# Waiting on SyncE for the first w1 of an expert to land before the next expert's weights are sent

## The reference, cut to what matters

```python
x = attention(r, k, v, w, u)                 # 1536 rows of 384
for layer in (0, 1):                          # two mixtures of experts, E = 8, F = 1024
    logits = x @ w_gate (+ bias by modality in layer 0)
    e_idx  = argmax(logits)                   # one expert to a row
    gate   = softmax(logits) at e_idx
    for e in range(8):
        rows   = (e_idx == e)                 # layer 1: at most capacity = 384 of them
        out[rows] = gate[rows] * (relu(x[rows] @ w1[e]) @ w2[e])
    x = out                                   # w1[e]: 384 x 1024, w2[e]: 1024 x 384, float32
```

## Time and profile before

| what | us |
|---|---|
| median of 3 runs (394.46 to 395.70) | 395.65 |
| the profiled execution: time | 396.4 |
| the profiled execution: span | 394.3 |
| TensorE matmuls busy (3406) | 366.7 |
| VectorE busy | 209.6 |
| ScalarE busy | 133.0 |
| GpSimd busy | 184.5 |

### The profile page before, as it was taken

One profiled execution on the slowest core, in us unless ns is written; L12 is line 12 of the kernel. 1 busy time (PEld: TensorE's weight loads), 2 busy tenths in 40 slices (PEclk: granted clock), 3 DMA queues, 4 the chain that ended last, 5 costly groups with the idle time before them and its releaser, 6 DMA issues.

```text
span 394.3 us, 10784 instructions
## 1 busy us (share of the span) xinstructions
PE 366.7 (93%) x3406; PEld 356.9 (91%) x3407; DVE 209.6 (53%) x539; ACT 133.0 (34%) x230; POOL 184.5 (47%) x303
## 2 busy tenths in 40 slices
PE   4689999988999999999999999879999999999990
PEld 4579999977899999999999999769999999999990
DVE  4356666689688655555555577474214454244210
ACT  2447554410544222222222252105215555255220
POOL 6798999815455532323232334152434524444311
PEclk9999999998999999999999999699999999999996
DMA  6898774146999511111111321139349998492000
GB/s 128 142 353 185 164 161 100 40 129 169 402 405 404 215 40 40 40 40 40 40 40 40 112 114 40 13 82 403 122 153 350 317 327 299 136 345 98 27 23 17
DMA packets 68238, 62.08 MB, mean 157 GB/s; under 512 B 45493, under 2 KB 61028, under 8 KB 68080
## 3 DMA queue, kind: packets, MB, share of 16 engines
q1 hardware_dynamic: 63904, 51.26, 40.9%
q0 software_dynamic: 3744, 10.23, 7.9%
q10 hardware_dynamic: 560, 0.21, 0.2%
HBM read 52.85 MB, written 10.14 MB: 160 GB/s over the span
## 4 chain that ended last, share of the span: by engine, by line
PE 82%; DMA 6%; SPq 4%; DVE 3%; issue 2%; ACT 1%; POOL 1%; ACTq 0%; POOLq 0%; DVEq 0%
PE p_h L1203 35%; PE p_o L1225 28%; DMA w_sb<-in_moe_w 3%; PE p_sc L1118 3%; SPq L406 3%; PE p_x L1090 3%; PE p_xt L1180 2%; PE p_y L1100 2%; PE p_y L1106 2%; DMA w_raw<-in_moe_w 2%; PE p_kv L1081 1%; PE p_kt L1068 1%; PE p_rt L1072 1%; PE p_o L1050 1%; DMA xg<-x_rows,src_idx 1%
## 5 line engine op out<-in xcount | busy, mean ns | idle before, releaser
L1203 PE MATMUL p_h<-xT,w_sb 128*128 128x128 f32 x1296 | 149.3, 275 | 1.6 <-ACT xT L670 1.0
L1203 PEld LDWEIGHTS p_h<-xT,w_sb 128*128 128x128 f32 x1296 | 148.2, 192 | 2.3 <-issue 1.3
L982 DVE SCALAR_TENSOR_TENSOR h_lo<-p_h,h_hi 128x512 fp32r<-128x512 f32 x54 | 37.4, 692 | 78.9 <-ACT h_hi L753 77.8
L999 DVE CUSTOM_DVE_ANT_0 lg_prod<-y_row,wg_all 128x384 f32<-128x384 f32 x112 | 55.8, 554 | 41.9 <-ACT y_row L763 41.7
L1225 PE MATMUL p_o<-w_hi,h_hi 128*128 x216 | 75.4, 349 | 0.0
L1225 PE MATMUL p_o<-w_lo,h_hi 128*128 x216 | 73.1, 339 | 0.0
L1225 PE MATMUL p_o<-w_hi,h_lo 128*128 x216 | 73.0, 338 | 0.0
L753 ACT ACTIVATE h_hi<-p_h 128x512 fp32r<-128x512 f32 x54 | 32.3, 598 | 112.2 <-PE p_h L1203 112.2
L580 POOL TENSOR_TENSOR dst_mark<-zeros 128x1 f32<-128x1 f32 x54 | 15.7, 290 | 105.8 <-DVE y_row L999 68.6
L839 DVE TENSOR_TENSOR w_lo<-w_raw,w_hi 128x1024 fp32r<-128x1024 f32 x36 | 42.0, 1221 | 7.8 <-ACT w_hi L670 7.8
L580 POOL TENSOR_TENSOR src_mark<-zeros 128x1 f32<-128x1 f32 x54 | 18.8, 348 | 49.1 <-PE p_xt L1180 33.9
(11 more groups left out here) (183 smaller groups left out, 408.9 us busy)
## 6 DMA issues: line engine op xcount, KB each, us to landing
w_raw<-in_moe_w SPq DMA_DIRECT2D x12, 1536.0 KB, 9.7
w_sb<-in_moe_w SPq DMA_DIRECT2D x12, 1536.0 KB, 9.5
k_raw<-in_k SPq DMA_DIRECT2D x12, 192.0 KB, 3.2
r_raw<-in_r SPq DMA_DIRECT2D x12, 192.0 KB, 3.6
v_raw<-in_v SPq DMA_DIRECT2D x12, 192.0 KB, 3.8
x_rows<-x_rows SPq DMA_DIRECT2D x12, 192.0 KB, 1.9
out<-zeros SPq DMA_DIRECT2D x1, 2304.0 KB, 15.6
wg_all<-in_moe_w_gate_by_expert SPq DMA_DIRECT2D x1, 1536.0 KB, 6.6
```

The lines of the kernel that those rows point to most:

```text
L982: stt(h_lo[:, at, :], p_h[n][:, :, :], 0.0, h_hi[:, at, :].bitcast(F32), ALU.max, ALU.subtract).then_inc(h_ready[layer], 1)
L999: last = nv.tensor_tensor_reduce(out=lg_prod[:, n, :], in0=y_row[par][:, 0:DM], in1=wg2_all[:, e, :], op0=ALU.mult, op1=ALU.add, scale=1.0 ...
L1203: last = mm(p_h[half][:, f, :], w1_sb[place][:, c, col:col + P], xT[:, c, :], start=(c == 0), stop=(c == DC - 1))
```

## The change

In the branch `free < 1`, after w1 has been sent, SyncE waits until the semaphore of that place, `w1_loaded[place]`, has reached 16, which is the count that the first load ever into this place leaves when it has landed. Nothing else differs.

```diff
@@ -469,6 +469,7 @@
 
                                 expert_w2(place, read_layer, read_e)
                             expert_w1(place, read_layer, read_e)
+                            sp.wait_ge(w1_loaded[place], 16)
                         with sp.If(free > 0):
                             sp.wait_ge(w2_ready, NPC * (n - 1))
                             expert_w2(place, read_layer, read_e)
```

## The result

| | us |
|---|---|
| before, median of 4 runs (394.46 to 395.70) | 395.24 |
| changed, median of 4 runs (399.35 to 402.50) | 400.74 |
| ratio, 95% interval | 1.0121, 1.009 to 1.0153 |
| changed, profiled execution: time, span | 399.35, 397.3 |

The changed kernel is slower by 1.2%, some 4.8 us (3.6 to 6.0); the two medians themselves lie 5.5 us apart. The time lies in the range of the prediction, above its point of 398.9, and near rival A's 400.3.

What follows compares the result with a forecast made beforehand. TensorE, busy 366.7 of 394.3 us, was taken as the bound, so at most 0.7 us could be won. Forecast: median 395.65 + 3.2 us for tile 2's later start, clock loss 0, = 398.9 us; range 395.9 to 401.7.

Steps and rivals of the forecast that it cites:

- rival A: TensorE at tile 2: the forecast's wait plus idle time pulling the clock down, 1.4 us more, 400.3 us; chance 0.27.
- L (step d): Moment expert 2's w1 has landed in layer 0, releasing SyncE: stays at 107.7, so the 0.7 us aren't won.
- rival B: Shared queue: expert 2's w1 was slowed by loads behind it, so it lands at 105.4; 395.7 to 396.6 us; chance 0.18.
- (b): SyncE after release: expert 3's w2 goes out about 1.1 us later, w1 half a microsecond behind it.
- (c): Expert 3's two loads on idle DMA engines: 12.3 us from first issue to second landing, ends 11.0 and 13.3.
- (e): Expert 3's w1 lands at 121.1, 5.4 us later; less 2.2 us of room, tile 2's p_h starts 3.2 us later.
- The hole in the DMA rate: Sign to look for in the trace: a gap of about 2 us in the DMA rate after 107.7.
- (f): Expert 3's w2 lands about 6.8 us after issue, ScalarE waits 1.3 us; covered by tile 2's wait, cost 0.
- (g): Later loads: n = 3's w2 goes out near 110.6, lands at 125, wanted at 127.5; covered, as are those after.
- (h): TensorE's clock after 3.2 us idle before tile 2: loss taken as 0 in the forecast, 1.7 us as bound.
- C: Rival at layer 0's first tiles: faster by 0.7 us, 394.95, if both experts' w1 land early enough; chance 0.07.
- D: Rival: expert 3's pair and expert 4's w2 share the DMA engines evenly, delaying tile 2 some 4 to 6 us; chance 0.05.

Runs made afterwards that it cites:

- swap: Kernel before, but for n = 1 in layer 0 SyncE sends expert 2's w1 ahead of its w2, no wait added; ratio to before 1.0061.
- again3: The changed kernel run again unchanged, third repeat; ratio to before 1.0101.
- wait_w2: The changed kernel, but SyncE waits for expert 2's w2 instead of its w1; ratio to before 0.9976.
- hold_w1: Kernel before, with the wait for expert 2's w1 placed after sending expert 3's w2, before expert 3's w1; ratio to before 1.0019.
- again2: The changed kernel run again unchanged, second repeat; ratio to before 1.0147.
- again: The changed kernel run again unchanged, first repeat; ratio to before 1.0098.
- fill2: Second run of the changed kernel with 50 small filler matmuls on TensorE after tile 1 of layer 0; ratio to before 1.0067.
- fill: The changed kernel plus 50 small filler matmuls on TensorE after tile 1 of layer 0, within its wait; ratio to before 1.0085.
- wait_high6: The changed kernel, but SyncE is released when ScalarE has done the third piece of expert 2's w2; ratio to before 1.0136, 2 executions.

## Why the prediction was right, and where its size was off

**L (step d) held**, and with it rival B fell: expert 2's w1 took 11.82 us from its issue (11.8 to 12.7 in the four profiles). The reading behind it, that a load isn't slowed by one behind it on SyncE's queue and that some engines run ahead while the last one finishes, is borne out by swap and by the changed kernel, where 0.04 MB were left for the last 1.9 us. On B the prediction is not consistent: with 11.0 us for the pair its own sum puts tile 2 at 117.5, 0.4 us earlier than 117.89, where it writes 0; its "middle, 395.9" goes with the -0.4.

**SyncE's branches (b)**: 1.1 us was taken, 1.2 us is measured. **The pair (c)**: 12.3 us was taken; it was 12.1 in the first profile (110.50 to 122.56), and 11.5 to 11.6 in the other three. **The sum (e)**: 3.2 us later was forecast; the first profile has 3.2, the four together 2.7 to 3.6 (tile 2's start, from the issue of expert 2's w2), and executions with the filler give 3.1. The hole in the DMA rate was larger than the "about 2 us" that was to be looked for: 1.9 us before the landing and 3.7 behind it. It cost the sum nothing, as (c) counts from the issue.

**(f)** ScalarE waited 2.2 us for expert 3's w2, not 1.3, because this load took 7.6 us rather than 6.8; it was covered by the wait for w1, as said. **(g)** was off in a detail that cost nothing: the w2 of expert 4 went out 3.0 us after that of expert 3, not 1.8 (108.8 to 110.6), since the issue of the w1 between them took 0.9 us by itself; neither ScalarE nor TensorE had a further wait.

**(h) is the term that was mis-sized.** The forecast took 0 for the clock and gave 0.40 to that, 0.27 to rival A with 1.4 us. The runs show A's mechanism in two of four profiles of the changed kernel, at 1.6 and 2.9 us, and 1.3 us (0.3 to 2.4) in the mean of whole executions. The changed kernel's mean is 4.5 us above before, 3.1 for the wait and 1.3 for the clock, which lies at A's 4.65 rather than at the forecast's 3.25. The range held because it had been drawn to A's bound. The error was to treat the clock as a yes or no for the kernel; the profiles show it one way in two executions and the other way in two, so that a share of it belongs in the sum. The two rows, one with the loss and one without, said as much, and 0.27 x 1.4, or 0.4 us, is what the prediction's own chance would have put in. The bound of 1.7 us was too low as well: in again3 the clock was at 0.50 from 120 to 126 us, longer than the 4 us of that row.

**C** (faster) fell, as L didn't move and no pair after empty engines took less than 11.5 us. **D** (all three share, 4 to 6 us) fell too: expert 3's w2 landed 7.6 us after its issue, at 118.1 in the first profile, where D needs 10 to 11 us (108.8 to 119 or 120).

## What to carry to other kernels

A wait on the engine that feeds a DMA queue costs the time in which the DMA engines then have no work, less the room that the next load has. That time starts before the landing waited for, here 1.9 us, and ends behind the next issue, here 1.2 us to issue and 2.5 us until data flow at the full rate. A wait that ends with the landing is too late; one that ended 4.3 us before it (wait_w2), or that had another load queued behind (hold_w1), cost nothing. A hold between loads of one queue doesn't make the first land sooner: to have a load sooner, send it ahead of the others, and then look at who waits for those. Where a new idle time of some us on TensorE is forecast, a share of a clock loss behind it belongs in the sum.

## What the runs showed of the hardware that was not expected

The tiles run at two speeds at the same granted clock of 1.00, and one kernel shows both. In the chain, tile follows tile after 9.92 us in the kernel before and in ten of the others, again2 and again3 among them, and after 9.85 us in the changed kernel's first profile and in again. It can change within an execution: in fill2 tile 3's p_o takes 4.17 us as the two before it, and all behind it 4.24. The page of the first has 336 ns for a matmul of this group where that of before has 338:

```profile
L1226 PE MATMUL p_o<-w_hi,h_lo 128*128 x216 | 72.5, 336 | 0.0
```

At 24 tiles this is 1.7 us, and it explains why the span of the changed kernel's profile is only 3.0 us longer while tile 2 starts 4.8 us later (1.6 us of the attention's clock and 3.2 us of the wait). What sets it stays open; it isn't the chip alone, since fill, wait_w2 and hold_w1 ran on the chip of again.

The clock also fell in the attention in some executions and not in others: behind about 29 us in four of the thirteen profiles (the changed kernel's first, again2, wait_w2 and wait_high6). In these four expert 2's w2 was issued at 97.0 to 98.0 us, in the other nine at 94.4 to 95.9. The four are of both kinds, with the wait for w1 and with other waits, and nothing that was changed runs that early. Such differences are part of the scatter between executions, how large a part isn't shown; it is why the stage had to be read in the profiles.
